# The staging buffer of y at another place in SBUF, and the first six loads of weight sums issued in one go

## What is computed

```python
def _moe_ref(x, w1, w2, w3, w_out):
    h = np.maximum(np.maximum(x @ w1, x @ w2), x @ w3)
    return (h @ w_out).astype(np.float32)

def _moe2_ref(x, w_in, w_out):
    h = x @ w_in
    g = np.where(h >= 1, h, np.where(h <= -1, 0.0, (h + 1) ** 2 / 4))
    return (g @ w_out).astype(np.float32)

x = attention(q, k, v, mem_k, mem_v)        # 3072 tokens x 512
x = _moe_ref(x, w1, w2, w3, w_out)          # 512 -> 768 -> 512
return _moe2_ref(x, w_in, w_out)            # 512 -> 2048 -> 512
```

## Time and profile before

| | us |
|---|---|
| median of three runs (1015.46 to 1018.89) | 1015.54 |
| profiled execution: its time | 1018.02 |
| profiled execution: span, first to last instruction | 1016.2 |
| TensorE busy in the span | 990.2 (97%) |
| VectorE / ScalarE / POOL busy | 509.2 / 378.0 / 130.5 |
| weight-sum loads, issue to landing, median of 8 | 13.2 |
| y stores, issue to landing, median of 32 | 2.5 |

### The profile page before, as it was taken

The page is one execution under the profiler, slowest core; times in us unless marked ns, Lnnn a source line. Parts: engine busy times, 40 slices in busy tenths (PEclk is TensorE's granted clock), DMA queues, the critical chain, the costliest instruction groups (busy, mean ns, idle before and its releaser), DMA issues.

```text
span 1016.2 us, 22988 instructions
## 1 busy us (share of the span) xinstructions
PE 990.2 (97%) x9792; PEld 975.8 (96%) x9792; DVE 509.2 (50%) x1011; ACT 378.0 (37%) x645; POOL 130.5 (13%) x128
## 2 busy tenths in 40 slices
PE   5999999999999999999989999999999999999997
PEld 4999999999999999999989999999999999999997
DVE  4563534343343434332446566565655656566564
ACT  3342212122222222242435445454544545445453
POOL 1113306143320000062100000000000000000000
PEclk9999999999999999999999999999999999999999
DMA  9453545263635320065890102011020210102000
GB/s 362 168 208 118 195 176 211 97 257 110 215 134 188 105 84 2 32 186 157 302 319 22 43 22 63 13 49 41 21 55 6 62 41 21 41 21 62 0 22 22
DMA packets 41797, 108.01 MB, mean 106 GB/s; under 512 B 2816, under 2 KB 29440, under 8 KB 39680
## 3 DMA queue, kind: packets, MB, share of 16 engines
q1 hardware_dynamic: 27904, 79.70, 21.6%
q0 software_dynamic: 13824, 27.27, 9.0%
HBM read 73.40 MB, written 33.55 MB: 105 GB/s over the span
## 4 chain that ended last, share of the span: by engine, by line
PE 93%; DMA 4%; issue 1%; DVE 1%; ACT 0%; POOL 0%; DVEq 0%; POOLq 0%
PE mlp L449 20%; PE mlp L451 19%; PE mlp L450 19%; PE scores_ps L451 4%; PE scores_ps L450 4%; PE scores_ps L449 4%; PE attn_ps L449 4%; PE attn_ps L451 4%; PE attn_ps L450 4%; PE attn_ps L442 3%; DMA wc<-wc_scratch 3%; PE scores_ps L418 2%; DMA y_scratch<-y_stage 1%; PE trans_ps L451 1%; PE trans_ps L450 1%; PE trans_ps L449 1%
## 5 line engine op out<-in xcount | busy, mean ns | idle before, releaser
L449 PE MATMUL mlp<-x_hi,w_hi 128*128 128x384 f32 x576 | 197.6, 343 | 3.2 <-issue 3.2
L451 PE MATMUL mlp<-x_lo,w_hi 128*128 128x384 f32 x576 | 193.6, 336 | 0.0
L450 PE MATMUL mlp<-x_hi,w_lo 128*128 128x384 f32 x576 | 193.3, 336 | 0.0
L449 PE MATMUL mlp<-y,w_in_hi 128*128 128x256 f32 x576 | 163.9, 284 | 4.1 <-DMA wc<-wc_scratch 4.1
L450 PE MATMUL mlp<-y,w_in_lo 128*128 128x256 f32 x576 | 163.7, 284 | 0.0
L451 PE MATMUL mlp<-y,w_in_hi 128*128 128x256 f32 x576 | 163.7, 284 | 0.0
L449 PEld LDWEIGHTS mlp<-y,w_in_hi 128*128 128x128 f32 x576 | 111.3, 193 | 4.3 <-issue 4.3
L449 PEld LDWEIGHTS mlp<-x_hi,w_hi 128*128 128x128 f32 x576 | 108.7, 189 | 5.9 <-issue 4.1
L857 DVE SCALAR_TENSOR_TENSOR g_f<-g_f,mlp 128x512 f32<-128x512 f32 x72 | 49.5, 688 | 128.5 <-ACT g_f L700 128.5
L450 PEld LDWEIGHTS mlp<-y,w_in_lo 128*128 128x128 f32 x576 | 111.4, 193 | 0.0
L451 PEld LDWEIGHTS mlp<-y,w_in_hi 128*128 128x128 f32 x576 | 111.3, 193 | 0.0
(11 more groups left out here) (97 smaller groups left out, 2004.0 us busy)
## 6 DMA issues: line engine op xcount, KB each, us to landing
qk_raw<-qk_l SPq DMA_DIRECT2D x24, 768.0 KB, 8.1
wc_scratch<-stage_a SPq DMA_DIRECT2D x8, 1792.0 KB, 8.4
wc<-wc_scratch POOLq DMA_DIRECT2D x8, 1792.0 KB, 13.2
v_raw<-v_l SPq DMA_DIRECT2D x24, 512.0 KB, 4.2
y_scratch<-y_stage SPq DMA_DIRECT2D x32, 384.0 KB, 2.5
y<-y_scratch POOLq DMA_DIRECT2D x24, 512.0 KB, 4.9
stage_a<-w SPq DMA_DIRECT2D x6, 768.0 KB, 7.1
stage_b<-w_out SPq DMA_DIRECT2D x8, 512.0 KB, 7.3
```

What stands on the lines that cost most here:

```text
L449: pe.matmul(out_ap, a_hi, b_hi, start=first, stop=False, skip_group_check=beside)
L450: pe.matmul(out_ap, a_lo, b_hi, start=False, stop=False, skip_group_check=beside)
L451: return pe.matmul(out_ap, a_hi, b_lo, start=False, stop=last, skip_group_check=beside)
```

## The change

`y_stage` is laid right behind `x1_lo` and no longer behind `h_max`. There it lies under `wc[6]`, and under nothing that the second half writes earlier. `w_out1`, `h_hi`, `h_lo`, `h_part` and `h_max` move up by its size. The wait of `raw_high` in unit 1 goes, loads 0 to 5 are issued one after the other, and the wait for all four stores moves behind `load_y(1)`, ahead of load 6.

```diff
@@ buffers
         x1_lo = sbuf(phase_a, "x1_lo", [KD, TT], F32R)
+        y_stage = sbuf(phase_a, "y_stage", [2, 2, TT], F32R)
...
-        y_stage = sbuf(phase_a, "y_stage", [2, 2, TT], F32R)
         phase_a.close()
@@ POOL
             pool.wait_ge(mlp_done, TG * (TILES - 1) + L1G)
-            load_wc(0)
-            for d in range(2):
-                pool.wait_ge(y_stored[d], 16 * AHEAD + 32 * (TILES - 1) + 16)
-                load_wc(1 + d)
-            for s in y_stored:
-                pool.wait_ge(s, 16 * AHEAD + 32 * TILES)
-            for p in range(3, 6):
+            for p in range(6):
                 load_wc(p)
             pool.wait_ge(mlp_done, TG * TILES)
             load_y(1)
+            for s in y_stored:
+                pool.wait_ge(s, 16 * AHEAD + 32 * TILES)
             load_wc(6)
             load_wc(7)
@@ ScalarE, raw_high
                 act.wait_ge(g_done, g + 1)
-                if isinstance(g, int) and g < 2:
-                    if g == 1:
-
-                        act.wait_ge(y_stored[0], 16 * AHEAD + 32 * TILES)
-                        act.wait_ge(y_stored[1], 16 * AHEAD + 32 * TILES)
-                else:
+                if not isinstance(g, int) or g >= 2:
                     act.wait_ge(down_done, g - 1)
```

## The result

The changed kernel takes 1026.64 us (median of 6 runs, 1024.24 to 1027.43) and the kernel before 1015.97 (median of 6). The ratio is 1.0097, 95% interval 1.0081 to 1.0113: about 10 us slower. The profiled executions are 1027.43 and 1018.02, 9.4 us apart, with spans of 1025.6 and 1016.2.

What follows compares the result with a forecast made beforehand. TensorE is busy 97% of the span, so only its waits or slow running count. Loss 15.3 + 1.6 = 16.9 us, less gain 7.5, is 9.4 us slower: 1025 us, range 1021 to 1032.

Steps and rivals of the forecast that it cites:

- The gains: At the handover to the second half, two TensorE waits (1.66 and 4.26 us) and 1.6 us of clock go: 7.5 us.
- The stores: y stores in q1 beside the loads in q0 creep, one record from each queue in turn, at 28.8 records a us.
- Store 0: First y store of the last tile: issued at 476.4, lands at 492.0, so TensorE's first unit starts 8.7 us late.
- the first record: Start of store 0 in q1: its first record moves 4.2 us after issue.
- the last engine: End of store 0: the last engine finishes 2 us after the mean engine.
- Store 1: Second y store, behind store 0 in q1: another 9.4 us, landing at 501.4, 20 to 23 us after issue.
- TensorE: Second unit of the second half starts at 502.6, 15.3 us late, the first unit's lateness and slow clock included.
- The clock: Half clock on TensorE behind the long wait for the y copies: 1.6 us lost once more.
- What comes next: Loads 6 and 7 land at 522, TensorE wants them at 539: no wait, 17 us to spare.
- g of unit one: Its ramp on ScalarE begins at 502, its product is wanted near 511: costs nothing.
- the second rival: Long turns: each engine does its whole share of a load, then of a store; 3.4 us gain, 1012; chance 0.09.

Runs made afterwards that it cites:

- own slots: The changed kernel, with staging buffers of their own for y blocks d = 2 and 3 of the last tile: 1009.65 us, 0.9935 of the kernel before.

## Why the prediction was right, point by point

**The gains.** Both waits of the earlier trace rows are gone, and with them the half clock behind the second. The most to be gained was put at 7.5 us; with own slots 7.55 were gained.

**The stores.** q1 moves one record for each of q0: 173 to 171 in 481:487, 358 to 361 in 487:499. The rate was put at 28.8 a us; over 487:499 it is 29.8. Store 0 landed 13.6 us after issue. I had 15.6, and "14 to 17" as the sign of being right, so this is just outside. Two terms were too large: the first record came 3.5 us after issue and not 4.2 (q1's first 11 records are in 479:480), and the last engine was about 1 us behind the rest and not 2. Store 1 took 21.5 us, in the range of 20 to 23.

**TensorE.** The kernel after is about 0.35 us ahead on its clock at this place. Without a wait its second unit would have begun at 483.97 + 0.17 + 2.86 = 487.00; it began at 501.90, so 14.9 us late against 15.3 forecast.

**The clock.** This term was mis-sized. It was put at 1.6 us, from the 16 slow matmuls behind the wait in the kernel before. Here all 24 matmuls of the second unit are slow, from 501.90 to 507.18, and cost 5.28 less 2.86 = 2.4 us. The granted clock is at the 1.2 GHz level for the first unit (first line) and for the second (the others):

```profile
494.00:496.00 2.00, 2.00 (x11) 2.00 (x11) 0.00 (x0) 0.00 (x0) 0.00 (x0) 0.50 1.01 406
...
502.00:504.00 2.00, 2.00 (x10) 2.00 (x11) 1.44 (x4) 0.91 (x2) 0.00 (x0) 0.50 1.01 351
504.00:506.00 2.00, 2.00 (x11) 2.00 (x11) 1.37 (x4) 0.74 (x1) 0.00 (x0) 0.50 1.40 385
506.00:508.00 2.00, 2.00 (x14) 2.00 (x14) 0.00 (x0) 0.58 (x1) 0.00 (x0) 0.66 0.95 278
```

How many matmuls are slow after a wait is not the same each time, and neither the length of the wait nor a second wait close by explains it. The first unit of the changed kernel stands behind one wait of 6.63 us, after work at the full clock, and all its 24 matmuls are slow. With the six loads alone the like wait is 6.48 us, and the 16th matmul is at full speed again (0.28 us and not 0.41):

```profile
493.66 0.28 PE L443 MATMUL mlp<-y,w_in_hi 128*128 128x256 f32 x1
```

The 15 slow ones take 3.36 us where 15 x 0.119 is 1.79, so the clock cost 1.6 us there, and 2.4 here. Why it was the one or the other stays open.

Loss 14.9 + 2.4 = 17.3 us, less 7.5 is 9.8; the two profiled executions are 9.4 apart and the medians 10.7.

**What comes next.** Loads 6 and 7 were forecast for 522, wanted at 539. They were issued at 508.77 and 509.3 and took 7.7 and 12.5 us, so the last landed at 521.8, and TensorE did not wait for them. Nor did g of unit one cost anything.

**The rule of the Trainium skill.** "DMA: Bandwidth & Descriptors", in its section on queues, rings and completion order, lets an engine drain a packet of about 9 to 17 descriptors before it turns to its next queue. The traces of this case do not agree, if a record in them is a descriptor: they show turns of one record. The 361 to 358 above do not decide that alone. An engine has 9 records of a load (144 / 16) and 17 of a store (272 / 16), so turns of nine would give nearly the same sums over 12 us. The single microseconds decide. These are 480:481, 483:484 and 486:487 of the changed kernel:

```profile
q0 software_dynamic: 25, 0.36, 86.3%
q1 hardware_dynamic: 25, 0.04, 12.3%
...
q0 software_dynamic: 34, 0.30, 72.8%
q1 hardware_dynamic: 36, 0.06, 16.6%
...
q0 software_dynamic: 25, 0.36, 85.8%
q1 hardware_dynamic: 24, 0.04, 11.8%
```

The 16 engines are nearly in step: the 16 short semaphore records that end a load fall together, so that 483:484 and 488:489 have 34 and 39 records of q0, and the others from 480 on 25 to 32. With turns of nine, q1 would then move some 144 records in about a us and none in the next four (9 x 16 records of q0 at 32.3 a us, an estimate from the earlier trace rows). It moves 24 to 41 in every us from 480 to 489. With 3.5 KB records it moves 37 to 41 in every half us of 480:485. Had each engine done its whole share in a turn, the change would have gained 3.4 us, by the sum of the second rival. The measurement decides here.

**What the sum did not say.** It was right in adding up, but the gain does not come in its parts: the place of y_stage alone is worth nothing, 1.0003, because the wait on load 7 stands behind it. Nor is it worth anything in the changed kernel: the six loads alone, with raw_high's wait kept, give 1.0092 against 1.0097. What it is worth where the last loads come early and the first two stores are quick, no run tells: in those runs the wait is gone.

## What to carry to other kernels

In these runs a small store beside a queue of large loads paid one of the loads' records for each of its own, and took 13.6 us where 2.5 is usual: count its rows, not its bytes. Before you issue loads early, look for the small transfers in the other queue whose landing frees a buffer, and give those a slot of their own, a head start, or shorter records beside them; three runs here did one each, and all turned a loss of 10 us into a gain of 5 to 8. And a pause in a hand-written order may be what keeps the other queue quick, so take pauses out one by one and not all at once.

## What the runs showed that I had not expected

- Rows that were contiguous on both sides stayed one record when the access pattern cut them in four: 13824 records of q0 over the span in both. Only another layout in DRAM made them shorter, and then q0 had 16896.
- Shorter records cost q0 little. Alone it moved 3.25 MB in 497:505 with 3.5 KB records, 0.406 a us, where 14 KB records gave 4.63 in 502:513, 0.421; no wait of TensorE came of it. Loads 6 and 7 were issued 11 us earlier than in the changed kernel, since the y stores that gate them were in by 497 (POOL's row; in the changed kernel it stands at 508.77):

```profile
497.52 1.50 POOL L371 DMA_DIRECT2D wc<-wc_scratch  x2 [11.94 <-DMA y_scratch<-y_stage]
```

- POOL's issue of a load in four pieces takes 0.75 us where one with joined rows takes 0.54 (1.50 for two here, 1.08 for two in the changed kernel).
